# The folded tile's swapped maxima and sums: from SBUF to two free columns of its PSUM bank

## What is computed

```python
# batch 4, 8 heads, seq 576, head_dim 64, block 64
scores = (q @ k.T) / 8
scores = where(pos_q // 64 >= pos_k // 64, scores, -1e9)
scores = scores - max(scores, axis=-1)
attn = exp(scores)
attn = attn / (sum(attn, axis=-1) + 1e-9)
x = attn @ v                              # heads joined: 2304 tokens x 512
h = x @ moe_w_in                          # 512 -> 2048
g = where(h >= 1, h, where(h <= -1, 0, (h + 1) ** 2 / 4))
x = g @ moe_w_out                         # 2048 -> 512
h = x @ moe2_w_in
out = (h * cos(h)) @ moe2_w_out
```

## Time and profile before

| | before |
|---|---|
| median of 3 runs (lowest, highest) | 1058.15 us (1056.0, 1058.56) |
| profiled execution, its own time | 1056.57 us |
| its span, first to last instruction | 1054.8 us |
| PE busy | 990.4 us, 94% of the span |
| DVE busy | 699.2 us, 66% |
| ACT busy | 582.1 us, 55% |
| POOL busy | 416.8 us, 40% |

### The profile page before, as it was taken

How to read it: one execution, slowest core, us unless ns; L and a number is a source line. 1 busy time by engine, 2 the same in 40 slices (tenths; PEclk the granted TensorE clock), 3 DMA queues, 4 the chain that set the end, 5 groups by cost and what they waited for, 6 DMA issues and landing times.

```text
span 1054.8 us, 19545 instructions
## 1 busy us (share of the span) xinstructions
PE 990.4 (94%) x7296; PEld 935.5 (89%) x7296; DVE 699.2 (66%) x1613; ACT 582.1 (55%) x1232; POOL 416.8 (40%) x446
## 2 busy tenths in 40 slices
PE   5689999998998999999999999999999999999998
PEld 4589998898898898999899999899999999999996
DVE  5677776877777877778763258665655656556564
ACT  5667766665655655656653247544454444544443
POOL 4468755554545454545442222222222222222221
PEclk9689999999999999999999999999999999999999
DMA  5334322311221221221201026110101101011000
GB/s 164 101 110 162 99 67 78 100 54 51 74 73 51 71 76 51 72 74 51 77 21 41 21 100 200 41 40 0 40 0 40 40 0 40 0 40 40 0 21 21
DMA packets 30886, 63.31 MB, mean 60 GB/s; under 512 B 3680, under 2 KB 11872, under 8 KB 30816
## 3 DMA queue, kind: packets, MB, share of 16 engines
q1 hardware_dynamic: 29664, 58.21, 17.4%
q10 hardware_dynamic: 1152, 4.19, 1.0%
HBM read 52.95 MB, written 9.44 MB: 59 GB/s over the span
## 4 chain that ended last, share of the span: by engine, by line
PE 67%; DVE 19%; ACT 7%; issue 5%; DMA 1%; ACTq 0%; POOL 0%; POOLq 0%; DVEq 0%
PE hidden L1235 29%; PE acc L1254 17%; PE acc L1268 9%; PE heads_out L1158 4%; PE scores L1111 4%; DVE stats L888 2%; DVE q_parts L859 2%; DVE pt_lo L910 2%; PE turned L1127 2%; ACT probs L687 2%; DVE work L978 1%; DVE stats L882 1%; DVE stats L878 1%; DVE work L983 1%; DVE wout_lo L958 1%
## 5 line engine op out<-in xcount | busy, mean ns | idle before, releaser
L616 POOL TENSOR_TENSOR g_lo<-work,g_hi 128x512 fp32r<-128x512 f32 x144 | 187.4, 1302 | 434.5 <-ACT g_hi L784 433.8
L1235 PE MATMUL hidden<-x_hi,win_lo 128*128 128x256 f32 x1128 | 315.0, 279 | 9.8 <-DVE pt_lo L910 4.6
L1235 PE MATMUL hidden<-x_hi,win_hi 128*128 128x256 f32 x1128 | 319.4, 283 | 1.2 <-DVE work L983 1.1
L1235 PE MATMUL hidden<-x_lo,win_hi 128*128 128x256 f32 x1128 | 313.5, 278 | 0.0
L1235 PEld LDWEIGHTS hidden<-x_hi,win_lo 128*128 128x128 f32 x1128 | 212.6, 188 | 12.9 <-DVE pt_lo L910 6.6
L1235 PEld LDWEIGHTS hidden<-x_hi,win_hi 128*128 128x128 f32 x1128 | 212.8, 189 | 5.2 <-DVE work L983 1.3
L1235 PEld LDWEIGHTS hidden<-x_lo,win_hi 128*128 128x128 f32 x1128 | 213.1, 189 | 3.6
L1268 PE MATMUL acc<-g_hi,wout_lo 128*128 128x256 f32 x576 | 162.9, 283 | 15.2 <-DVE pt_lo L910 15.2
L1268 PE MATMUL acc<-g_hi,wout_hi 128*128 128x256 f32 x576 | 167.3, 290 | 2.3 <-ACT y_stage L767 2.3
L586 POOL TENSOR_SCALAR probs<-probs,stats 128x320 f32<-128x320 f32 (+2 forms) x160 | 98.8, 621 | 160.8 <-DVE stats L905 160.1
L1268 PE MATMUL acc<-g_lo,wout_hi 128*128 128x256 f32 x576 | 160.6, 279 | 0.0
(11 more groups left out here) (118 smaller groups left out, 1928.0 us busy)
## 6 DMA issues: line engine op xcount, KB each, us to landing
qk_raw<-qk_late SPq DMA_DIRECT2D x32, 480.0 KB, 3.4
qk_raw<-qk_early SPq DMA_DIRECT2D x32, 256.0 KB, 2.6
v_raw<-v_late SPq DMA_DIRECT2D x32, 160.0 KB, 3.4
x_raw<-x_scratch SPq DMA_DIRECT2D x9, 512.0 KB, 3.4
out<-y_stage SPq DMA_DIRECT2D x36, 128.0 KB, 2.4
x_raw<-w_in SPq DMA_DIRECT2D x8, 512.0 KB, 3.6
y_stage<-w_out SPq DMA_DIRECT2D x8, 512.0 KB, 3.6
x_scratch<-y_stage ACTq DMA_DIRECT2D x8, 512.0 KB, 2.8
```

What stands on the lines that cost most here:

```text
L616: nc.gpsimd.tensor_tensor(g_lo[:, m % G_RING, :], work[:, m % 2, :], g_hi[:, m % G_RING, :], ALU.subtract).then_inc(g_lo_made, 1)
L1235: last = nc.tensor.matmul(into, w[:, p, c, half * P:(half + 1) * P], x[:, c, :], start=(i == 0), stop=(i == len(products) - 1))
```

## The change

The two spare columns leave SBUF. `swap_of(n, which)` gives column 320 or 321 of the bank that holds tile 4's scores, and the copies write there. The minimum and the sum then read one input from PSUM and one from SBUF, where both inputs were in SBUF; the PSUM one is put first. The sum's spare column keeps the bank in use until `inverse` is through, so where `score` emits a wait on the exponential of a late item it would now wait on the inverse. Item 32 follows an early item, and for items 33 to 63 `banks_seen` is true as before, so no such wait is emitted in either kernel. The order of each engine's instructions is the same in both.

```diff
-        stats = sb("stats", [P, 3 * 15 + 2], F32)
+        stats = sb("stats", [P, 3 * 15], F32)
         neg_max, row_sum, row_inv = stats[:, 0:15], stats[:, 15:30], stats[:, 30:45]
-        max_swap, sum_swap = stats[:, 45:46], stats[:, 46:47]
...
+        def swap_of(n, which):
+
+            return scores[:, n % 2, FOLD + which:FOLD + which + 1]
...
+                max_swap = swap_of(n, 0)
                 m = n - HEADS + 1
                 nc.vector.tensor_reduce(out=top, in_=bank, axis=AX_X, op=ALU.max, negate=True).then_inc(half_max_made, 1)
                 dve.wait_ge(half_max_made, m)
...
                 dve.wait_ge(max_swapped, 2 * m)
-                nc.vector.tensor_tensor(top, top, max_swap[:, :], ALU.min).then_inc(max_made, 1)
+                nc.vector.tensor_tensor(top, max_swap, top, ALU.min).then_inc(max_made, 1)
...
+                    sum_swap = swap_of(n, 1)
                     for to, source in ((0, BLOCK), (BLOCK, 0)):
                         nc.vector.tensor_copy(sum_swap[to:to + BLOCK, :],
                                               row_sum[source:source + BLOCK, col:col + 1]).then_inc(sum_swapped, 1)
                     dve.wait_ge(sum_swapped, 2 * (n - HEADS + 1))
-                    nc.vector.scalar_tensor_tensor(out=sums, in0=sums, scalar=EPS, in1=sum_swap[:, :], op0=ALU.add,
+                    nc.vector.scalar_tensor_tensor(out=sums, in0=sum_swap, scalar=EPS, in1=sums, op0=ALU.add,
                                                    op1=ALU.add).then_inc(sum_guarded, 1)
...
                 elif e == 1 and n > ALONE and not banks_seen(n):
-                    pe.wait_ge(exp_made, first_tile(n))
+
+                    if late(n - 1):
+                        pe.wait_ge(inv_made, first_tile(n))
+                    else:
+                        pe.wait_ge(exp_made, first_tile(n))
```

## The result

| | before | after |
|---|---|---|
| median (lowest, highest) | 1058.36 us (1056.0, 1059.72), 4 runs | 1040.36 us (1039.99, 1041.69), 4 runs |
| profiled execution, own time | 1056.57 us | 1041.69 us |
| its span | 1054.8 us | 1039.9 us |
| PE, DVE, ACT, POOL busy | 990.4, 699.2, 582.1, 416.8 us | 987.5, 682.5, 584.0, 417.2 us |

The changed kernel takes 0.9834 of the time before (95% interval 0.9815 to 0.9854), 18.0 us less by the medians. A later set of five runs of the same kernel gave 0.9839 (0.9824 to 0.9854), 16.2 us by its medians. The forecast was 13.0 us less. All times in this document are of executions at a granted clock of 0.98 to 0.99; one execution of psum_second was granted 0.565, took 1629.35 us and is left out.

The account below looks back on a forecast made before the run. PE was taken as the bound, idle 25.2 us in the late items, 21.1 waiting for L910. PE's gain of 14.4 us less 1.4 gave 13.0, so 1058.15 - 13.0 = 1045.1 us; range 1040 to 1053.

Parts of the forecast that it names:

- What holds L888: Maxima's join on DVE: an instruction with both inputs in SBUF is held while POOL works in SBUF; 749 ns, unheld 158.
- DVE's savings: Both joins: 18.9 us saved in L888 and 2.7 in L902, together 21.6 us of DVE; the copies cost nothing extra.
- the rival on PSUM: Joins and copies: PSUM is dear for short instructions, up to 53 ns each, gain about 7 us, 1051 us; chance 0.05.
- estimate from the Trainium skill: Both joins: a PSUM source costs 65 ns more each, 4.1 us of DVE, saving 17.5 us in place of 21.6.
- smaller-of-two rule: Per late item, PE gains the smaller of DVE's saving and PE's wait for L910: 14.4 us over 32 items.
- the two deductions: Late items: 0.7 us lost where PE waited longer, 0.7 us where items newly meet L592 or L616; 14.4 becomes 13.0.
- The other item that the prediction worked through: Item at 329 us: L888 gives 0.92 us, PE had waited 2.39, so PE gets 0.92.
- The wait that moves to L859: Query remainder on DVE comes earlier and meets POOL's value remainder L592, ending 0.41 us after it; mean at most 0.8 us.
- the gain given back: At L859: POOL's normalisation goes first, each item behind L579 brings at most 0.24 us; 7 us gained, 1051; chance 0.13.
- the slower one: At L859: it falls behind an L616 of 1.29 us, +0.62 us an item; 1061.5 us if half do; chance 0.05.
- what of it reaches PE: From L888 to L910: DVE and ACT move forward together, PE gains up to its wait for L910, the rest becomes slack.
- POOL's 320-column normalisation: On POOL in late items: it should stay stretched, since it stands behind L859; unheld 0.53 us.

Follow-up runs that it names:

- psum_second: The changed kernel with each join's two inputs in the old order, SBUF column first and PSUM column second: 1041.5 us, ratio 0.9845.
- pointer: The kernel before, all in SBUF, with both joins taking the spare column as a per-partition scalar operand: 1040.62 us, ratio 0.9845.
- pool_late: The kernel before, with POOL making late items' key and value remainders behind the folded tile's normalisation instead of ahead: 1075.02 us, ratio 1.0152.
- held_extra: The changed kernel plus a one-column minimum with two SBUF inputs ahead of the maxima's join, no other tensor moved: 1063.2 us, ratio 1.0049.
- free_extra: The changed kernel plus a one-column minimum with one PSUM input ahead of the maxima's join, no other tensor moved: 1041.33 us, ratio 0.9844.
- pad_32: The changed kernel plus an unused tensor of 32 bytes a partition ahead of x_raw and what follows, no instruction added: 1057.01 us, ratio 0.9989.
- extra_psum: The changed kernel plus a minimum with one PSUM input ahead of the maxima's join, its output a new tensor behind ident: 1056.61 us, ratio 0.9988.
- extra_sbuf: The changed kernel plus a minimum with two SBUF inputs ahead of the maxima's join, its output a new tensor behind ident: 1078.25 us, ratio 1.0195.

## Why the prediction was right, point by point

**What holds L888.** Right, and shown from three sides: by taking one of the two SBUF inputs away in two different ways (the change, pointer), by moving POOL (pool_late), and by putting a held instruction back (held_extra against free_extra).

**DVE's savings.** The two joins went from 24.0 + 7.8 us to 5.1 + 5.0, 21.7 us against the 21.6 of the sum. The four copies cost 160 ns instead of 149, so PSUM as a target costs 11 ns here, 1.4 us of DVE in all, where the sum had nothing. That is far from the 53 ns that the rival on PSUM took as its bound. PSUM as a source costs these joins nothing: 158 ns as before, 156 as second input. The prediction's estimate from the Trainium skill, "VectorE: DVE Perf Modes", section on the TRN2 errata, 65 ns more for each join, isn't borne out by these instructions.

**Who gets it.** PE's waits for the remainder fell by 12.0 us, against 14.4 from the smaller-of-two rule and 13.0 after the two deductions. So 2.4 us should have been taken off and not 1.4. One item in detail, the same one as in the earlier trace rows and now at 313 us: DVE, then POOL.

```profile
313.21 0.16 DVE L893 TENSOR_TENSOR stats<-scores,stats 128x1 f32<-128x1 f32 x1
...
314.83 0.67 DVE L862 SCALAR_TENSOR_TENSOR q_parts<-qk_raw,q_parts 64x384 fp32r<-64x384 f32 x1
```

```profile
312.82 1.43 POOL L582 TENSOR_TENSOR k_lo<-qk_raw,k_hi 128x576 fp32r<-128x576 f32 x1
314.20 0.88 POOL L595 TENSOR_TENSOR v_parts<-v_raw,v_parts 128x320 fp32r<-128x320 f32 x1
315.06 0.85 POOL L589 TENSOR_SCALAR probs<-probs,stats 128x320 f32<-128x320 f32 x1
```

The join starts inside L582 and isn't held. L862 starts in L595 (to 315.08), ends at 315.50, 0.42 us behind it, and POOL's L589 gives way: the forecast had 0.41 us. PE doesn't wait in this item at all, where it had waited 0.50 us.

The other item that the prediction worked through, at 329 us in the earlier trace rows, came out less well. The forecast gave PE 0.92 us of its wait of 2.39; the wait is 1.81 now, 0.58 less. The tokens' remainder, a DVE instruction with two SBUF inputs that the prediction didn't look at, now runs into POOL's value remainder (324.25 to 325.12) and takes 0.36 us more. Two of them are merged in each line, before and after:

```profile
331.66 1.29 DVE L972 TENSOR_TENSOR x_lo<-x_raw,x_hi 128x512 fp32r<-128x512 f32 x2 [0.60 <-ACT x_hi L760]
```

```profile
324.62 1.65 DVE L978 TENSOR_TENSOR x_lo<-x_raw,x_hi 128x512 fp32r<-128x512 f32 x2 [0.61 <-ACT x_hi L763]
```

**The wait that moves to L859.** 15 of 31 query remainders are held now (7 before), each by one POOL instruction and for 0.35 us in the mean, 5.2 us in all, which is 0.17 us over the 31. The group's mean, 726 ns, is inside the 0.8 that was given, so both rivals about this place (the gain given back, and the slower one, which needed a mean wait over 0.67 us) didn't come about. POOL's instruction is the value remainder in 11 of them, as the forecast had it, the activations' remainder in 2, and the keys' remainder and a normalisation in one each.

**The term that was missing.** The forecast of 13.0 was 3.9 short of the 16.9 us in the stretch. The wait that the sum counted fell by 1.0 us less than forecast, so pieces that the sum didn't have brought 4.9 us. The two errors have opposite signs, and that 1.0 us of them cancelled is luck. Three pieces of the fall can be read. First, the waits for DVE, 12.0 us. Second, PE's idle time for other releasers fell from 4.0 to 2.1 us; 1.2 of it is in the first item, where PE waits for ACT to empty `acc`, and ACT stands behind the exponential that waits for the join. Third, the first matmul behind a wait takes 0.39 us, as in the last line of the earlier trace rows, where its neighbours take 0.28, and the matmul behind it starts 0.22 us later where others of this size follow after 0.11. All of PE's waits count here, whatever their length; they fell from 35 to 15, and an estimate of 20 x 0.11 is 2.2 us. That makes 16.1 of 16.9. What the last 0.8 us are stays open. The step of the prediction that was off is thus "what of it reaches PE": it took PE's recorded idle time for one releaser as the whole cost of a wait, and it counted L859 alone as what is held next. The other two pieces are read from two traces and not tested by a run.

**The numbers.** The predicted time was 1045.0 us with 1040.0 to 1053.0 as the range, and 1040.36 lies at its lower edge. The mechanism was right, and the gain was put too low by a quarter. POOL's 320-column normalisation stayed stretched as forecast (783 ns in the mean, 804 before, 530 unheld), while the copies weren't left at 149 ns and PE's waits for DVE ended at 9.1 us, not 7.

## What to carry to other kernels

A tiny instruction with a large and uneven duration is a wait in disguise: set its end against the other engines' ends before believing its cost. If it is a two-input DVE instruction in SBUF beside a busy POOL, one input from PSUM (158 ns) or as a scalar operand (214 ns) freed it in this kernel, and whatever two-input instruction comes next should be freed in the same edit where it can be, since it inherits the wait (the sums' join 243 to 443 ns here, and about 4 us of the gain). In an experiment that adds a tensor, keep every other tensor where it was, or the control will measure the move.

## What the runs showed of the hardware that was not expected

- **Where matmul operands start.** 32 bytes more ahead of x_raw, x_hi, x_lo, work, g_hi and g_lo cost 15.7 us of 1041, with matmuls of 256 columns at 281 to 282 ns in place of 277 to 278. By the tensors' declared sizes, each start rounded up to 32 bytes, these six start at multiples of 64 bytes in the kernels without the shift and at odd multiples of 32 with it; the traces give no addresses. That a start at 64 is the rule, and which of the operands needs it, wasn't tried; the runs show one shift of 32 bytes, three times (pad_32 against free_extra 15.7 us in one set; across two sets, extra_psum against free_extra 15.3 us and extra_sbuf against held_extra 15.1 us). The change shrinks `stats` by two columns, but this moved no tensor: pointer, which keeps the 47 columns, has the same time.
- **A scalar operand is not a second input.** The scalar form in SBUF was never held in 64 instructions (212 to 218 ns), beside a POOL as busy as before.
- **A waiting DVE instruction goes first.** Where it already waited when POOL's instruction ended, it went ahead of the next one in POOL's queue, in the item shown above as in the earlier trace rows. All 15 held query remainders of the changed kernel end 0.40 to 0.42 us after the end of the POOL instruction that they met.
